# VectorE's 32x32 transposes in place of TensorE's, in a fused attention, dense and expert kernel

## The reference

```python
# 1. decayed linear attention: B=2, H=8, S=768, D=64, in blocks of 64; x is [1536, 512]
intra = ((q_b @ k_b.T) * Dmask) @ v_b;  inter = (q_b * lam_pow) @ kv_state
x = heads of (intra + inter), side by side
# 2. dense: w_in [512, 2048], w_out [2048, 512]
h = x @ w_in;  x2 = np.maximum(0.01 * h, h) @ w_out
# 3. experts: 8 of them, w1 [512, 1024], w2 [1024, 512]; one per token
logits = x2 @ w_gate + modality_bias[modality_id]
e_idx = argmax(logits);  gate_w = softmax(logits)[e_idx]
out[tokens of e] = gate_w * (np.maximum(x2[tokens of e] @ w1[e], 0) @ w2[e])
```

## Time and profile before

| | |
|---|---|
| median of 3 runs | 517.16 us (517.04 to 517.98) |
| the profiled execution | 516.76 us, span 515.0 us, TensorE clock granted 0.997 |
| chain that ended last | PE 79%, DMA 9%, DVE 5%, issue 3% |
| DMA moved | 53.16 MB, mean 103 GB/s |

### The profile page before, as it was taken

How to read it: one execution, slowest core, us unless ns; L and a number is a source line. 1 busy time by engine, 2 the same in 40 slices (tenths; PEclk the granted TensorE clock), 3 DMA queues, 4 the chain that set the end, 5 groups by cost and what they waited for, 6 DMA issues and landing times.

```text
span 515.0 us, 8856 instructions
## 1 busy us (share of the span) xinstructions
PE 495.7 (96%) x2974; PEld 402.6 (78%) x2975; DVE 192.2 (37%) x412; ACT 181.2 (35%) x309; POOL 205.4 (40%) x221
## 2 busy tenths in 40 slices
PE   7899999999999999999999999999989999999993
PEld 6778888888878888887888888888778787888850
DVE  4533333343334622221462266647322283222110
ACT  1233343333334344344434456522222282222210
POOL 3874654654315347533334664504120162212101
PEclk9999999999999999999999999999999999999998
DMA  6955434332020170001800000121288738311100
GB/s 200 408 231 164 159 130 159 109 107 44 1 83 1 44 283 0 0 0 54 323 31 1 2 0 0 40 84 41 71 243 259 242 103 265 96 47 41 41 1 20
DMA packets 23242, 53.16 MB, mean 103 GB/s; under 512 B 8119, under 2 KB 9791, under 8 KB 23216
## 3 DMA queue, kind: packets, MB, share of 16 engines
q1 hardware_dynamic: 17792, 46.03, 25.8%
q0 software_dynamic: 2544, 6.77, 4.1%
q10 hardware_dynamic: 2880, 0.02, 0.3%
HBM read 46.40 MB, written 6.61 MB: 103 GB/s over the span
## 4 chain that ended last, share of the span: by engine, by line
PE 79%; DMA 9%; DVE 5%; issue 3%; ACT 1%; ACTq 1%; POOL 0%; DVEq 0%; SPq 0%; POOLq 0%
PE psum L1360 9%; PE psum L1368 8%; PE psum L1370 8%; PE psum L1369 8%; PE psum L1362 8%; PE psum L1361 8%; DMA ids_s<-slots_d 3%; PE psum L1449 3%; PE psum L1451 2%; PE psum L1450 2%; PE psum L1429 2%; PE psum L1323 2%; PE psum L1431 2%; PE psum L1430 2%; PE psum L1318 2%
## 5 line engine op out<-in xcount | busy, mean ns | idle before, releaser
L572 POOL TENSOR_TENSOR wi_lo<-wd_raw,wi_hi 128x512 fp32r<-128x512 f32 x48 | 62.1, 1294 | 145.2 <-ACT wi_hi L729 145.1
L1360 PE MATMUL psum<-xT,wi_lo 128*128 128x512 f32 x192 | 77.3, 402 | 0.0
L1368 PE MATMUL psum<-wo_hi,act_lo 128*128 128x512 f32 x192 | 75.7, 394 | 1.3 <-DVE act_lo L987 1.3
L1362 PE MATMUL psum<-xT,wi_hi 128*128 128x512 f32 x192 | 75.0, 391 | 0.0
L1361 PE MATMUL psum<-xT,wi_hi 128*128 128x512 f32 x192 | 74.9, 390 | 0.0
L1370 PE MATMUL psum<-wo_hi,act_hi 128*128 128x512 f32 x192 | 74.8, 390 | 0.0
L1369 PE MATMUL psum<-wo_lo,act_hi 128*128 128x512 f32 x192 | 74.7, 389 | 0.0
L984 DVE SCALAR_TENSOR_TENSOR act_f<-psum,act_f 128x512 f32<-128x512 f32 x48 | 33.1, 690 | 97.2 <-ACT act_f L747 96.7
L577 POOL TENSOR_TENSOR wo_lo<-wd_raw,wo_hi 128x512 fp32r<-128x512 f32 x48 | 61.9, 1290 | 2.7 <-ACT wo_hi L734 2.7
L747 ACT ACTIVATE act_f<-psum 128x512 f32<-128x512 f32 x48 | 28.7, 597 | 97.4 <-PE psum L1362 94.2
L987 DVE TENSOR_TENSOR act_lo<-act_f,act_hi 128x512 fp32r<-128x512 f32 x48 | 33.8, 705 | 33.6 <-ACT act_hi L749 33.6
(11 more groups left out here) (204 smaller groups left out, 758.1 us busy)
## 6 DMA issues: line engine op xcount, KB each, us to landing
we_raw<-w_exp SPq DMA_DIRECT2D x40, 512.0 KB, 4.7
wd_raw<-w_dense SPq DMA_DIRECT2D x16, 512.0 KB, 5.6
qk_in<-attn_qk SPq DMA_DIRECT2D x10, 512.0 KB, 3.4
kv_in<-attn_kv SPq DMA_DIRECT2D x10, 512.0 KB, 3.5
x_d<-x_sb SPq DMA_DIRECT2D x12, 256.0 KB, 2.4
qk_more<-attn_qk SPq DMA_DIRECT2D x2, 512.0 KB, 6.7
kv_more<-attn_kv SPq DMA_DIRECT2D x2, 512.0 KB, 7.4
decay_mask<-pow_d SPq DMA_DIRECT2D x2, 256.0 KB, 3.7
```

The lines of the kernel that those rows point to most:

```text
L572: nc.gpsimd.tensor_tensor(wi_lo[:, r, :], dense_raw(f, 0), wi_hi[:, r, :].bitcast(F32), ALU.subtract).then_inc(s_wil, 1)
L1360: nc.tensor.matmul(h, w_lo, hi, start=(c == 0), stop=False)
L1362: mm = nc.tensor.matmul(h, w_hi, hi, start=False, stop=(c == DC - 1))
L1368: nc.tensor.matmul(bank(ACC + i), lo, wo_hi[:, r, :], start=first, stop=False)
```

## The change

The second dense layer swaps its operands: the weights are stationary and the activations move, so each of the four banks holds 128 features x 512 tokens. ACT copies the banks to `x2T`, which the gate multiplication uses as it is. The gate weights are padded to 32 columns, and each of the four feature chunks has its own group of 32 PE columns (`logit_parts`); four small matmuls with a 0/1 matrix `of_expert` add the four parts and bring tokens to partitions (`logits`). For the store, DVE transposes 32x32 squares straight from PSUM (`turn_x2`) to `x2_r`; partition a*32+j then holds, for tokens j of each group of 32, the features a*32 to a*32+31 of every chunk. SP stores 512-byte pieces, four DMAs of 512 pieces; a token's row in DRAM is four such pieces. A tile is gathered by four indirect DMAs of 128 pieces, at ids times four plus a quarter number (POOL arithmetic in place of a copy), with ids loaded by four DMAs of 4-byte elements. DVE then transposes 32x32 squares of `xg` to PSUM (`turn_rows`), and `rows` and `rows_lo` go on from there. The mixed rows go the same way. All PE transposes of x2 rows and of gathered rows are gone; those of hidden activations stay. On DVE, `rows_lo(2)` and `hid(1, 1)` now stand before the arithmetic of `m_tab`; on ACT, the ids of tile PRE + 1 are loaded before `hid(2, 0)`, two steps earlier.

```diff
-        x2_d = nc.dram_tensor("x2_d", [TOK + 1, DM], F32).ap()
+        x2_d = nc.dram_tensor("x2_d", [(TOK + 1) * QS, P], F32).ap()
+        x2_rows = x2_d.rearrange("(t a) c -> t (a c)", a=QS)
...
+                sp.wait_ge(s_xr, DC * (t + 1))
+                for a in range(QS):
+                    sp.dma_start(x2_d[t * BLK * QS:(t + 1) * BLK * QS, :].rearrange("(b j a) n -> a j b n", a=QS, j=QR)[a],
+                                 x2_r[a * QR:(a + 1) * QR].rearrange("p b c i -> p b (c i)")).then_inc(s_x2st, 16)
...
+                for g in range(QS):
+                    pool.indirect_dma_start(out=xg[:, g * P:(g + 1) * P], out_offset=None, in_=x2_d[0:SURE * QS, :],
+                                            in_offset=bass.IndirectOffsetOnAxis(
+                                                ap=at_pre4[:, t * QS + g:t * QS + g + 1].bitcast(U32), axis=0),
+                                            bounds_check=SURE * QS - 1, oob_is_err=False).then_inc(s_gat, 16)
...
+            pool.wait_ge(s_idp, 16 + LOADS)
+            nc.gpsimd.tensor_scalar(at_pre4[:], at_pre[:], float(QS), quarter[:], ALU.mult, ALU.add).then_inc(s_chain, 1)
+            pool.wait_ge(s_chain, 9)
             gather_early(0)
...
-                nc.gpsimd.tensor_copy(ids_g[:], ids_n[:]).then_inc(s_idc, 1)
+                nc.gpsimd.tensor_scalar(ids_g[:], ids_n[:], float(QS), quarter[:], ALU.mult, ALU.add).then_inc(s_idc, 1)
...
+            for q in range(MIX):
+                pool.indirect_dma_start(out=xg_m[:, q, :], out_offset=None, in_=x2_d,
+                                        in_offset=bass.IndirectOffsetOnAxis(ap=at_m4[:, q:q + 1].bitcast(U32), axis=0)
+                                        ).then_inc(s_mgat, 16)
...
-                for i in range(TPB):
+                if t > 0:
+                    act.wait_ge(s_lgt, t)
+                for c in range(DC):
                     if tail:
-                        act.wait_ge(s_tile, i + 1)
-                    n = TPB * t + i
-                    if n >= X2R:
-                        act.wait_ge(s_x2t, n - X2R + 1)
-                        act.wait_ge(s_x2st[n % X2R], 16 * (n // X2R))
-                    nc.scalar.activation(x2_sb[:, n % X2R, :], bank(ACC + i), ACT.Copy).then_inc(s_x2, 1)
+                        act.wait_ge(s_tile, c + 1)
+                    nc.scalar.activation(x2T[:, c, :], bank(ACC + c), ACT.Copy).then_inc(s_x2, 1)
...
+            def load_rows(t):
+                slot = act.value_load(tab[0:1, bass.ds(SB_ + t, 1)], min_val=0, max_val=SLOTS - P)
+                with nc.allow_non_contiguous_dma(reason="one id each"):
+                    for a in range(QS):
+                        act.dma_start(ids_n[a * QR:(a + 1) * QR, :],
+                                      slots_d[bass.ds(slot, P), 0:1].rearrange("(g j) b -> j (g b)", j=QR)).then_inc(s_ids, 16)
...
-            load_ids(ids_n, PRE, s_ids)
+            load_rows(PRE)
             hid(1, 1)
             relu(2, 0)
+            act.wait_ge(s_idc, PRE + 1)
+            load_rows(PRE + 1)
             hid(2, 0)
             relu(2, 1)
             rows(3)
...
+            def turn_x2(t):
+
+                if t > 0:
+                    dve.wait_ge(s_x2st, LOADS * t)
+                for c in range(DC):
+                    dve.wait_ge(s_x2, DC * t + c + 1)
+                    nc.vector.transpose(x2_r[:, :, c, :], bank(ACC + c).rearrange("p (b i) -> p b i", i=QR)).then_inc(s_xr, 1)
+
+            def logit_parts(t):
+                dve.wait_ge(s_lgt, t + 1)
+                nc.vector.tensor_copy(lgT[:], logit_bank(t)).then_inc(s_lgc, 1)
...
+            def turn_rows(t):
+                dve.wait_ge(s_gat, LOADS * t + LOADS)
+                dve.sem_inc(s_pass, 1)
+                dve.wait_ge(s_exl, t)
+                nc.vector.transpose(bank(T_PS).rearrange("p (c g j) -> p g c j", c=DC, g=QS),
+                                    xg[:].rearrange("p (g c i) -> p g c i", g=QS, c=DC)).then_inc(s_et, 1)
...
-                    for i in range(3):
-                        turned(t - 1, i)
-                        leaky(n0 + i, i % 2)
-                    turned(t - 1, 3)
+                    turn_x2(t - 1)
+                    leaky(n0, 0)
+                    logit_parts(t - 1)
+                    leaky(n0 + 1, 1)
+                    leaky(n0 + 2, 0)
                     route(t - 1)
...
+            turn_rows(0)
             rows_lo(0)
-            for i in range(TPB):
-                turned(BLOCKS - 1, i)
+            turn_x2(BLOCKS - 1)
+            logit_parts(BLOCKS - 1)
+            turn_rows(1)
             route(BLOCKS - 1)
             hid(0, 0)
             gates(BLOCKS - 1)
             rows_lo(1)
             slots(BLOCKS - 1)
             hid(0, 1)
+            turn_rows(2)
...
+            rows_lo(2)
+            hid(1, 1)
...
+                turn_rows(t + 2)
...
-            def sums(r, i, first=False, last=False):
-
-                hi, lo = (x[:, r, i * P:(i + 1) * P] for x in (act_hi, act_lo))
-                nc.tensor.matmul(bank(ACC + i), lo, wo_hi[:, r, :], start=first, stop=False)
-                nc.tensor.matmul(bank(ACC + i), hi, wo_lo[:, r, :], start=False, stop=False)
-                return nc.tensor.matmul(bank(ACC + i), hi, wo_hi[:, r, :], start=False, stop=last)
+            def sums(r, c, first=False, last=False):
+
+                hi, lo = (w[:, r, c * P:(c + 1) * P] for w in (wo_hi, wo_lo))
+                nc.tensor.matmul(bank(ACC + c), hi, act_lo[:, r, :], start=first, stop=False)
+                nc.tensor.matmul(bank(ACC + c), lo, act_hi[:, r, :], start=False, stop=False)
+                return nc.tensor.matmul(bank(ACC + c), hi, act_hi[:, r, :], start=False, stop=last)
...
+            def logit_parts(t):
+
+                pe.wait_ge(s_x2, DC * (t + 1))
+                if t == BLOCKS - 1:
+                    pe.wait_ge(s_xr, DC * t + 2)
+                for c in range(DC):
+                    mm = nc.tensor.matmul(logit_bank(t)[c * QR:(c + 1) * QR, :], wg[:, c, :], x2T[:, c, :],
+                                          start=True, stop=True, skip_group_check=True)
+                mm.then_inc(s_lgt, 1)
+
+            def logits(t):
+                pe.wait_ge(s_lgc, t + 1)
                 for i in range(TPB):
...
+                    mm = nc.tensor.matmul(bank(MISC)[:, i * E:(i + 1) * E], lgT[:, i * P:(i + 1) * P], of_expert[:],
+                                          start=True, stop=True)
                 mm.then_inc(s_lg, 1)
...
-                    turn(t - 1, 0)
                     layer1(n0 + 1, 1, t)
-                    logits(t - 1, 0)
-                    turn(t - 1, 1)
-                    pe.wait_ge(s_x2, TPB * t)
+                    logit_parts(t - 1)
+                    pe.wait_ge(s_xr, DC * t)
                     layer2(n0, 0, first=True)
-                    logits(t - 1, 1)
-                    turn(t - 1, 2)
                     layer1(n0 + 2, 0, t)
-                    logits(t - 1, 2)
-                    turn(t - 1, 3)
+                    logits(t - 1)
...
-            transposes(0)
             pe.wait_ge(s_wol, n1)
             pe.wait_ge(s_gl, n1)
-            last_tile(0)
-            last_tile(1)
-            turn(t, 0)
-            last_tile(2)
-            turn(t, 1)
-            logits(t, 0)
-            last_tile(3)
-            turn(t, 2)
-            logits(t, 1)
+            for c in range(DC):
+                last_columns(c)
             pe.wait_ge(s_first, FC2)
             up(0, 0, 0, range(2))
-            turn(t, 3)
-            logits(t, 2)
+            logit_parts(t)
             up(0, 0, 0, range(2, DC))
-            logits(t, 3)
+            logits(t)
             up(0, 0, 1, range(2))
             turn_hidden(0, 0)
             up(0, 0, 1, range(2, DC))
-            transposes(1)
             ranks(BLOCKS - 1)
...
-                transposes(t + 2)
...
-                transposes(t + 1)
```

More of the change, by code:

```diff
@@ L499, in _ @@
                 sp.dma_start(ids_m[q * MR:(q + 1) * MR, :], slots_d[bass.ds(at, MR), :]).then_inc(s_mids, 16)
-            sp.wait_ge(s_gat, 16 * (PRE + 1))
+                with nc.allow_non_contiguous_dma(reason="one id each"):
+                    for a in range(QS):
+                        sp.dma_start(at_m[a * QR:(a + 1) * QR, q:q + 1], slots_d[bass.ds(at, MR), 0:1]).then_inc(s_mids, 16)
+            sp.wait_ge(s_gat, LOADS * (PRE + 1))
+            sp.wait_ge(s_ids, LOADS * (PRE + 1))
             with sp.Fori(KNOWN, whole + MIX) as o:
@@ L851, in _ @@
                 act.wait_ge(s_scat[i], 16 * CHUNKS // 2)
-            for i in range(X2R):
-                act.wait_ge(s_x2st[i], 16 * CHUNKS // X2R)
+            act.wait_ge(s_x2st, LOADS * BLOCKS)
             relu(1, 1)
@@ L964, in finish @@
                                         ALU.subtract).then_inc(s_xl, 1)
+            for a in range(QS):
+                nc.vector.memset(quarter[a * QR:(a + 1) * QR, :], float(a))
```

(14 more changed lines are left out.)

157 lines of the change are left out of this document (76 added, 81 removed).

## The result

The changed kernel took 521.19 us (median of 20 runs, 517.13 to 527.87); the kernel before, on the same chip, 516.93 (20 runs, 514.69 to 519.19). The ratio of the fast runs, which leaves out the changed kernel's two slow ones (527.7 and 527.9 us), is 1.0087, 95% interval 1.0063 to 1.011. I had forecast 507.0, range 500.5 to 514.5, and given 0.86 to faster. Its profiled execution took 522.88 us, span 521.0; the one of before 516.76, span 515.0.

The account below looks back on a forecast made before the run. TensorE, busy 495.7 of 515.0 us, was taken as the bound. Savings of 7.7 (blocks 1 and 2), 0.3 (tiles to down(7,0)), 1.9 (four later periods) and 0.3 (mixed rows) made 10.2: 507.0 us, range 500.5 to 514.5.

Parts of the forecast that it names:

- Blocks 1 and 2, 7.7: End of dense blocks 1 and 2: less router work and waiting, saving 4.4 and 3.3 us.
- B: Rival: DVE's 128x512 turns take 1.4 us, not 0.69, losing time at block ends; 514.4 us, chance 0.13.
- C: Rival: float32 gate matmuls in four column groups do not overlap, up to 11 us; 518 us, chance 0.04.
- A: Rival: gathers hide while expert weights stream, down(7,0) 5.6 us early; 501.7 us, chance 0.24 with the cases between.
- Block 3, 3.3: End of block 3: same instructions as block 2, so 3.3 us saved, counted in the tile stage.
- the wait for act_lo and wo_lo: Start of the tile stage: 1.1 us lost where wo_lo comes behind four gather issues instead of one.
- L: Time from a gather's first issue to last landing in loaded tiles: 8.9 us; from 12 the change loses.
- the stall at gather 5: Tile 5, while weights stream: rows land at 398.0, their turn should start at 394.0, a 4 us stall.
- hid(1,1): Start of the tile stage: 0.7 us lost where this hidden copy stands behind ACT's four id loads.
- PE gains there, up to the start of down(3,0): Start of the tile stage: gains less losses, taken as 5.5 us, bringing down(3,0) from 386.67 to 381.2.
- rival D: Tiles 5 to 9: quarter gathers serialise under load, slower; 527 us if L is 14 or more; chance 0.10.
- 0.3 are left: Tiles 5 to 7: late gathers and POOL's splits leave 0.3 of 5.5 us gained, down(7,0) at 437.6.

Follow-up runs that it names:

- turn_behind_route: Changed kernel with only VectorE's turn of tile 1's gathered rows moved behind the last block's routing and the first hidden copy; 520.02 us, ratio 1.0078.
- four_gathers: Against the changed dense part with whole-row gathers, TensorE turns and reordered expert weights: each gather split into four issues of 32 whole rows; 515.12 us, ratio 0.9999.

## Why the prediction was wrong, step by step

I had forecast 10.2 us off the span and it grew by 6.0, so 16.2 are missing: 12.3 up to the start of down(7,0), 3.4 behind POOL's last issue, 0.5 between.

- **Blocks 1 and 2, 7.7: right.** 7.5 measured. Gate matmuls of a block and their sums took 1.0 and 0.8 us, the wait of the earlier trace rows is gone, a turn of VectorE takes 0.68 to 0.73. Rivals B and C fall; so does A, since PE waited 3.55 us for gather 5's rows.
- **Block 3, 3.3: right, by difference.** Less the wait for act_lo and wo_lo, for which I had 1.1 us and which was 2.0, 7.5 + 3.3 - 2.0 = 8.8, the gain at T0. act_lo took 2.51 us instead of 0.69, beside POOL.
- **POOL's pitch (1.3), L (8.9, measured 8.6), the stall at gather 5 (4, measured 3.55), hid(1,1) (0.7, measured 0.44), gather 3 (1.0, measured 0.70), late periods (11.86, measured 11.85): right.**
- **"PE gains there, up to the start of down(3,0)": this step failed.** I had down(3,0) at 381.2 - 7.7 = 373.5 and it came at 380.77, 7.3 late. (The terms I listed for it add up to 5.7, not to 4.7 as I wrote; the 5.5 that I took hardly differs.) I followed gather 1 on POOL and PE and never asked what stands behind its turn on VectorE, though rival D names that very order. The routing does: 4.28 us, and 1.4 more by the half clock behind it. turn_behind_route removes it and shows why even this correction would not have saved the forecast. Slack won early is not kept: the next gather in DVE's order brings a wait of 2.15 us, and the wait for gather 5 ends at nearly the same time, 401.33 instead of 401.00.
- **Tiles 5 to 7, "0.3 are left": too kind.** down(7,0) should have come at 437.6 - 7.7 = 429.9 in the changed kernel's time and came at 442.23, 12.3 late. 7.3 of it had come about by down(3,0), 3.7 more by down(5,0) (412.33), 1.3 more by down(7,0). By cause: 4.3 and 0.9 from the tail, 1.25 where ScalarE's rows(4) stood behind its four id loads for tile 5, 3.8 by the clock; some 2 are left, of small differences in both directions. The waits for splits, hidden turn and scatter behind gather 5 were 5.3 where I had 4.9, so that chain was about right.
- **The clock: missing from the sum.** I priced a wait at its length. The three that I counted out (4.28, 2.90 and 3.55 us) cost 1.4, 1.6 and 2.4 us on top; in the changed kernel that is 3.8.
- **The end: missing, put at nothing without a reason.** 3.4 us behind POOL's last issue, with the number of indirect DMAs.
- **Rival D (slower, 527) had the sign, not the mechanism, and the place only in part.** I made it hang on L reaching 12 us, in tiles 5 to 9. L was 8.6, more than half of the 12.3 us had come about before tile 3, and the kernel is slower all the same. The rule on coalescing in "DMA: Bandwidth & Descriptors", section "Rules for kernel authors", of the Trainium skill did bear out here: 12.3 us from the number of indirect DMAs. The 7.8 more with 512-byte pieces come at the same number of DMAs and bytes. I had given rival D 0.10.
- **And a gain I undervalued.** Without the gathers' change the dense part brings 13 us, not 11: the four waits of 3.5 us together that the kernel before had are gone as well. One of them, 1.16 us for xe_lo, is what I had put down to rows_lo(2) going ahead of the mixed table; why the others went was not tried.

What stays open: why the span's end grows with the indirect DMAs executed, how the 7.8 us divide between small pieces, id arithmetic and issuing, and what the x2 stores beside gather 1 cost. The cost of the four id loads apart from the gain of VectorE's turns was not tried.

## What to carry to other kernels

When an operation moves to another engine, write down that engine's queue behind it and let each wait fall on everything in it; then do the same for every DMA that was split, with the issue time on the issuing engine counted for each tile, and ask which other transfers it now meets. In kernels like this one, price a wait of TensorE of about 3 us or more at its length plus 1.4 to 2.4 us for the slow matmuls behind it; for one of about 2 to 3 us allow for it. And when a change has two parts that meet in one buffer, look for a layout that lets the cheap part stand alone: here a reordering of weights in memory gave 502.9 us, where the whole change gave 521.2.

## What the runs showed of the hardware that I had not expected

- From 100 us on, up to the last work, the granted clock was 0.50 for 3 to 7 us behind each of the eight PE waits of 2.90 us or more in these traces (the longest 4.28), and never behind one under 1.8 us. Between the two it fell behind 8 of 17: 2.00 us at 326 in the changed kernel left it at 1.00, 1.97 us at 327 in turn_behind_route did not (0.50 from 329 to 331).
- VectorE's elementwise work can take far longer beside GpSimd's. Here act_lo runs over the end of a gather issue and the whole of a POOL subtraction (VectorE's and POOL's timeline of the changed kernel). Of its 38 executions from 100 us on 36 took 0.69 us; one at 290.66 that met 1.0 us of POOL's subtractions took 1.12. Which of issue and subtraction held this one up, no run separates:

```profile
323.30 2.51 DVE L1021 TENSOR_TENSOR act_lo<-act_f,act_hi 128x512 fp32r<-128x512 f32 x1 [0.70 <-ACT act_hi L779]
...
323.98 1.27 POOL L600 TENSOR_TENSOR wo_lo<-wd_raw,wo_hi 128x512 fp32r<-128x512 f32 x1
```

- An indirect DMA of 32 rows costs POOL 0.86 to 0.93 us as a rule (four_gathers), one of 128 rows 0.98 to 1.00 as a rule (before): almost all of it is per DMA, not per row.
- Each further indirect DMA lengthened the end of the span by about 0.08 us, and added 16 packets to POOL's queue, in the four kernels that have further ones (9, 39, 39 and 41).
